# First group of the scan: zero products moved beside the updates, a bank of its own for the fourth turned block, copies in pieces, key transfers in halves

## The reference, cut to what matters

```python
def _attn_ref(q, k, v, beta):              # 4 batches, 8 heads, 768 tokens, head size 48
    k_n = k / (norm(k) + 1e-06)
    state = zeros(B, H, D, D)
    for t in range(S):
        kt, vt, bt = k_n[:, :, t], v[:, :, t], beta[:, :, t]
        y[:, :, t] = q[:, :, t] @ state
        v_old = state^T kt
        state = state + bt * outer(kt, vt - v_old)
# x = y as (3072 tokens, 384)
# _moe_ref: softmax gate, 8 Sinkhorn rounds, 8 experts: out += P[:, e] * (relu(x @ w1[e]) @ w2[e])
# _moe2_ref: h = x @ w_in; (h * cos(h)) @ w_out
```

## Time and profile before

| | before |
|---|---|
| median of three runs | 2214.7 us |
| the profiled execution's own time | 2215.68 us |
| its span | 2213.9 us |
| mean granted TensorE clock | 0.985 |
| PE busy | 2169.7 us, 98% |
| DVE, ACT, POOL busy | 46%, 32%, 23% |

### The profile page before, as it was taken

The page is one execution under the profiler, slowest core; times in us unless marked ns, Lnnn a source line. Parts: engine busy times, 40 slices in busy tenths (PEclk is TensorE's granted clock), DMA queues, the critical chain, the costliest instruction groups (busy, mean ns, idle before and its releaser), DMA issues.

```text
span 2213.9 us, 41130 instructions
## 1 busy us (share of the span) xinstructions
PE 2169.7 (98%) x15885; PEld 1793.8 (81%) x15885; DVE 1019.6 (46%) x1724; ACT 702.7 (32%) x1197; POOL 507.2 (23%) x409
## 2 busy tenths in 40 slices
PE   8798999999999999999999999999999999999999
PEld 7777778888888888888888888888888888888887
DVE  8898726432322323223223232232322347777777
ACT  4655543111111111111111111111111237666665
POOL 1000010045332322323323233232332330000000
PEclk6899999999999999999999999999999999999999
DMA  5434332021111111111111101111111100000001
GB/s 140 121 91 119 104 117 74 24 54 43 29 33 29 29 40 36 32 30 28 33 28 28 47 28 33 28 30 32 28 35 42 29 24 15 15 15 15 0 15 71
DMA packets 83116, 97.74 MB, mean 44 GB/s; under 512 B 6848, under 2 KB 68608, under 8 KB 83008
## 3 DMA queue, kind: packets, MB, share of 16 engines
q1 hardware_dynamic: 83008, 96.18, 16.0%
HBM read 82.69 MB, written 8.75 MB: 41 GB/s over the span
## 4 chain that ended last, share of the span: by engine, by line
PE 91%; DVE 6%; issue 1%; ACT 1%; DMA 0%; SPq 0%; DVEq 0%; ACTq 0%
PE h L774 7%; PE h L776 7%; PE h L775 7%; PE p_h L774 7%; PE p_h L776 7%; PE p_h L775 7%; PE am_y L812 4%; PE am_y L813 4%; PE am_y L814 4%; PE cy_y_y L812 4%; PE cy_y_y L813 4%; PE cy_y_y L814 4%; PE o_y L812 2%; PE o_y L813 2%; PE state_y L814 2%; PE state_y L812 2%
## 5 line engine op out<-in xcount | busy, mean ns | idle before, releaser
L1384 POOL TENSOR_TENSOR acc<-acc,py 128x512 f32 (+1 forms) x252 | 324.1, 1318 | 746.2 <-DVE py L1732 746.2
L1244 ACT ACTIVATE hhi<-h 128x512 fp32r<-128x512 f32 x182 | 109.0, 599 | 769.7 <-PE h L776 769.7
L1695 DVE SCALAR_TENSOR_TENSOR hlo<-h,hhi 128x512 fp32r<-128x512 f32 x182 | 125.9, 692 | 473.5 <-ACT hhi L1244 473.5
L1695 DVE SCALAR_TENSOR_TENSOR hlo<-p_h,hhi 128x512 fp32r<-128x512 f32 x182 | 125.8, 691 | 404.3 <-ACT hhi L1244 404.3
L1346 POOL TENSOR_TENSOR wlo<-stage,whi (+1 forms) x114 | 146.8, 1289 | 630.1 <-ACT whi L1089 605.2
L774 PE MATMUL p_h<-xhi,whi 128*128 (+1 forms) x690 | 269.1, 390 | 0.6 <-DVE scr L1792 0.6
L774 PE MATMUL h<-xhi,whi 128*128 (+1 forms) x690 | 268.9, 390 | 0.0
L776 PE MATMUL h<-xhi,wlo 128*128 (+1 forms) x690 | 268.7, 389 | 0.0
L776 PE MATMUL p_h<-xhi,wlo 128*128 (+1 forms) x690 | 268.7, 389 | 0.0
L775 PE MATMUL p_h<-xlo,whi 128*128 (+1 forms) x690 | 268.6, 389 | 0.0
L775 PE MATMUL h<-xlo,whi 128*128 (+1 forms) x690 | 268.6, 389 | 0.0
(11 more groups left out here) (279 smaller groups left out, 3820.6 us busy)
## 6 DMA issues: line engine op xcount, KB each, us to landing
stage<-wcat SPq DMA_DIRECT2D x38, 768.0 KB, 4.4
pb<-p_scratch SPq DMA_DIRECT2D x84, 256.0 KB, 4.7
kq<-kqt SPq DMA_DIRECT2D x48, 192.0 KB, 3.5
v<-vrow SPq DMA_DIRECT2D x24, 192.0 KB, 3.7
kb<-krow SPq DMA_DIRECT2D x24, 192.0 KB, 3.8
acc<-yT SPq DMA_DIRECT2D x144, 32.0 KB, 2.3
kT<-kta SPq DMA_DIRECT2D x20, 192.0 KB, 4.3
acc<-y_scratch SPq DMA_DIRECT2D x5, 768.0 KB, 4.7
```

What stands on the lines that cost most here:

```text
L1244: act.activation(hhi[:, j, :], hps[j % 2][:, 0:TILE], ACT.Relu).then_inc(s["hhi_done"], 1)
L1384: pool.tensor_tensor(y, y, py[:, d, :], ALU.add).then_inc(s["added"], 1)
L1695: dve.scalar_tensor_tensor(out=hlo[:, j, :], in0=hps[j % 2][:, 0:TILE], scalar=0.0, in1=hhi[:, j, :].bitcast(F32), op0=ALU.max, op1=ALU.su ...
```

## The change: what it does

- **Zero products.** Before the scan: 14 in place of 6 ahead of the first joins, and 4 in place of 2 ahead of the first turned blocks. In the steps they stood in `beside_residual`, ahead of the wait for R; now they stand behind `beside_update`, after the next step's query products: 4 in (0,0), 2 in (0,1), 3 in (0,2), 2 in (0,3), 2 in (1,0), 3 in (1,1), none in (1,2). Four more stand in (0,0) between `joins(3)` and `turned(3)`.
- **Own bank.** `turned(3)` writes `h_ps` in place of `o_ps`, no longer waits for `fixed(2)`, and moves from step (0,1) to the end of (0,0). `joined(3)` on ACT moves ahead of `first_scatter(1)`.
- **ACT order in the first group.** `first_scatter(2)` moves behind the outputs of (0,1). The key copies `products(3, ...)` move from ahead of the update copy W to behind the outputs. `extract(2)`, four pieces in one go before, is spread: one piece after (0,1), one in (0,2) before the state, two after its outputs.
- **SP.** The first half of `wraw` stays in (0,0); the second moves from (0,1) to (1,2), and its ACT split from (0,3) to (1,3). The two halves of kT for group 4, both issued in (0,2) before, are issued in (0,2) and (0,3); those for group 5, both in (1,0) before, in (1,0) and (1,1). `move_y`, which runs in odd steps, stands ahead of them.
- **DVE.** Before the scan, the mask copies and `masked(0)` move ahead of `fixed(0)`.

```diff
-UNREAD = {(0, 1): 3, (0, 2): 3, (0, 3): 3, (1, 0): 3, (1, 1): 3, (1, 2): 3}
+UNREAD = {(0, 0): 4, (0, 1): 2, (0, 2): 3, (0, 3): 2, (1, 0): 2, (1, 1): 3}
@@ SP, in the loop over the steps, behind move_y
-                if g == 0 and c < 2:
-                    load_w(0, c, wraw)
-                if (g, c) in ((0, 2), (1, 0)):
-                    for part in range(2):
-                        load_kT(AHEAD + 1 + g, part)
+                if (g, c) in ((0, 0), (1, 2)):
+                    load_w(0, g, wraw)
+                if (g, c) in ((0, 2), (0, 3)):
+                    load_kT(AHEAD + 1, c - 2)
+                if (g, c) in ((1, 0), (1, 1)):
+                    load_kT(AHEAD + 2, c)
@@ PE, turned(c)
-            if c > 0:
+            if c in (1, 2):
                 pe.wait_ge(a["zx_fixed"], c)
+            bank = h_ps if c == STEPS - 1 else o_ps
@@ PE, beside_residual
             if (g, c) == (0, 1):
-                turned(3)
                 first_merge(2)
-            if (g, c) in UNREAD:
-                pe.wait_ge(a["m_evac"], {(0, 1): 2, (0, 2): 4, (0, 3): 4, (1, 0): 6}.get((g, c), 8))
-                unread(UNREAD[g, c], am_ps[1 if (g, c) == (0, 3) else 0])
@@ PE, step
             query_products(i + 1)
             beside_update(g, c)
+            if (g, c) in UNREAD:
+                bank = {(0, 0): o_ps, (0, 1): h_ps, (0, 3): am_ps[1]}.get((g, c), am_ps[0])
+                if g == 0 and c < 2:
+                    pe.wait_ge(a["zx_fixed"], 2 + 2 * c)
+                else:
+                    pe.wait_ge(a["m_evac"], 4 if g == 0 else 6)
+                unread(UNREAD[g, c], bank)
...
                 turned(2)
                 joins(3)
+                unread(4, am_ps[1])
+                turned(3)
@@ PE, before the scan
-        unread(6, state_ps)
+        unread(14, state_ps)
...
-        unread(2, state_ps)
+        unread(4, state_ps)
@@ ACT
-                if (g, c) in KEYS_BESIDE:
+                if (g, c) in KEYS_BESIDE and g > 0:
                     ... products(...) ahead of updates(g, c)
...
                     second_merged(2)
-                    first_scatter(2)
                     first_merged(3)
+                elif (g, c) == (0, 2):
+                    extract(2, 1, 2)
@@ ACT, behind the outputs
                     second_merged(1)
+                    joined(3)
                     first_scatter(1)
-                    joined(3)
                 if (g, c) == (0, 1):
+                    first_scatter(2)
                     second_merged(3)
                     first_scatter(3)
+                    extract(2, 0, 1)
+                if (g, c) in KEYS_BESIDE and g == 0:
+                    ... products(...)
+                if (g, c) == (0, 2):
+                    extract(2, 2, 4)
-                if c == 1 and far:
+                if c == 1 and far and g > 0:
                     extract(g + 2)
-                if g == 0 and c == 3:
+                if g == 1 and c == 3:
                     for chunk in range(NT // 2, NT):
                         split_hi(0, chunk, 0, 1, wraw)
@@ DVE, before the scan
-        fixed(0)
-        leaf_start(1)
         ... mask copies
         masked(0)
+        fixed(0)
+        leaf_start(1)
         fixed(1)
```

More of the change, by code:

```diff
@@ L529, in turned @@
             pe.wait_ge(a["join_evac"], c + 1)
-            if c > 0:
+            if c in (1, 2):
                 pe.wait_ge(a["zx_fixed"], c)
+            bank = h_ps if c == STEPS - 1 else o_ps
             for n in range(HEADS):
                 for b in range(2):
-                    mm = pe.matmul(rows(o_ps, b)[:, n * HL:(n + 1) * HL], rows(join, b)[:, c * HEADS + n, :],
+                    mm = pe.matmul(rows(bank, b)[:, n * HL:(n + 1) * HL], rows(join, b)[:, c * HEADS + n, :],
                                    rows(z_x, b)[:, c * HEADS + n, HL:L], start=True, stop=True)
@@ L1180, in _ @@
                     second_merged(1)
+                    joined(3)
                     first_scatter(1)
-                    joined(3)
                 if (g, c) == (0, 1):
+                    first_scatter(2)
                     second_merged(3)
                     first_scatter(3)
+                    extract(2, 0, 1)
+                if (g, c) in KEYS_BESIDE and g == 0:
+                    key_group, m = KEYS_BESIDE[g, c]
+                    products(key_group, 2 * m)
+                    products(key_group, 2 * m + 1)
+                if (g, c) == (0, 2):
+                    extract(2, 2, 4)
                 if (g, c) in KEYS_AFTER:
@@ L1509, in fixed @@
             units = slice(c * HEADS, (c + 1) * HEADS)
+            bank = h_ps if c == STEPS - 1 else o_ps
             z = z_x[:, units, HL:L]
-            dve.tensor_tensor(z, z, o_ps[:, 0:HEADS * HL].rearrange("p (n i) -> p n i", i=HL), ALU.subtract).then_inc(a["zx_fixed"], 1)
+            dve.tensor_tensor(z, z, bank[:, 0:HEADS * HL].rearrange("p (n i) -> p n i", i=HL), ALU.subtract).then_inc(a["zx_fixed"], 1)
             dve.wait_ge(a["zx_fixed"], c + 1)
```

## The result

The changed kernel took 2230.7 us in the median (2228.7 to 2231.3, 4 runs) beside 2216.1 for the kernel before (4 runs): a ratio of 1.0062, 95% interval 1.0045 to 1.0080. Later, beside other runs of the kernel before, it took 2228.7 us (4 runs), ratio 1.0060 (1.0040 to 1.0080). So it is slower by some 13.5 us, where 6.3 were forecast and the range ended at +10.8 (2225.5). The forecast time, 2221.0, was counted from the first three runs of the kernel before (median 2214.7); with the fourth its median is 2216.1, so 1.4 us of the distance to 2230.7 lie in that base.

A forecast was written before the change was run, and what follows sets the result against it. PE is busy 98% of the span after the scan, DVE bounds up to R(0,2). +0.8 + 0 - 3.9 + 0.3 + 8.8 + 0.3 = +6.3 us on 2215.7, less 1.0 to the median: 2221.0 us; range 2210.5 to 2225.5.

The forecast's parts named there:

- Part 5: Step (1,2): key half (5,1), issued behind the y moves, lands late and PE waits; +8.8 us (+5 to +9.5).
- Rival (b): SP's queue: the y moves let key half (5,1) through in time, so step (1,2) loses nothing; 2209.4 us, chance 0.17.
- Part 3: R(0,3) to end of (0,3): W starts when the weight split ends, issue stall gone; -3.9 us (-0.5 to -4.5).
- Part 4: End of (0,3) to end of (1,1): late key half (4,1) lands when needed; 0 us (-0.5 to +1.5), plus 0.3 for the clock.
- Part 1: Up to R(0,2): zero products delay R(0,1), DVE's two idles go, clock halfway; +0.8 us (-3.6 to +2.7).
- Part 2: R(0,2) to R(0,3): the 4.2 us wait on W goes or shrinks but DVE's chain decides; 0 us (-0.5 to +0.5).
- Rival (c): Clock low all through (0,0) and (0,1), issue stall of (0,3) half kept; +10 us, 2224.8 us, chance 0.18.
- rival (a): Clock holds at full from 26 us, so the stretch up to R(0,2) gains 3.6; +1.9 us, 2216.6 us, chance 0.23.

The follow-up runs named there:

- E9: The kernel before with only the second key half of group 5 moved, to (1,1) behind the y moves; 2226.35 us, ratio 1.0038.
- E4: The kernel before with ACT's new order in the first group alone; 2219.4 us, ratio 1.0007.
- E15: The changed kernel with keys, zero products and second weight half as before; 2216.9 us, ratio 0.9997.
- E6: The changed kernel with keys and zero products as before; 2216.5 us, ratio 0.9991.
- E2: The kernel before with only the key halves of groups 4 and 5 spread as in the change, behind the y moves; 2228.8 us, ratio 1.0048.
- E10: The kernel before with only the second key half of group 4 moved, to (0,3) behind the y moves; 2219.15 us, ratio 1.0002.
- E3: The kernel before with all the zero products of the change and nothing else; 2220.8 us, ratio 1.0015.
- E5: The changed kernel with both key halves of a group issued together in (0,2) and (1,0), as before; 2221.0 us, ratio 1.0011.
- E13: The kernel before with the change's early zero products alone, up to (0,1); 2218.0 us, ratio 1.0000.
- E14: The kernel before with the change's late zero products alone, from (0,2) on; 2218.0 us, ratio 1.0002.

## Why the prediction was wrong in size and right in direction

**Part 5, right.** The forecast's 8.8 + 0.3 stands against 10.0 in the profiles and 8.4 in E9's times. Within it two terms were off and nearly cancel. The half came sooner (products at +14.0 us, forecast +15.3), since the moves started 0.7 us earlier and took 8.04 us and not 8.9. What followed took longer (9.4 us from the first key product, forecast 7.5): PE's list behind the keys runs in series and at the lower clock, where I had W on ACT as last. Rival (b) is refuted by E9: the half does not pass the moves. One reading of the forecast was wrong and did no harm: the half was not "in place long ahead before". In the kernel before its two DMAs were issued only by 106.1 us, with the half ahead of them, for which PE already waited a little (1.4 us in the second execution):

```profile
109.05 0.27 PE L471 MATMUL h<-kT 48*64 48x64 f32 x2 [0.40 <-DMA kT<-kta]
```

The Trainium skill, DMA: Bandwidth & Descriptors, section "Issuing engines are not separate DMA queues", says the time to start a DMA is usually small beside the DMA. In the two steps where a key half stood behind them, the twelve small moves took 8.0 to 10.4 us to issue, 0.7 to 0.9 each, and landed in 2.0 to 2.8 in the median: for them the time to issue is the larger of the two for the series, and a third of the DMA for each.

**Part 3, the failed step, 5.1 of the 6.9 us between the table's 13.2 and the forecast 6.3.** It said: "W starts when the weight split ends, R + 4.1 (78.97 + 1.65 - 76.54), + 0.5, then 2.7 us for lines 698 to 709". W did start at R + 4.0, but was not last. I had not priced PE's own list from R to line 698 in its new form at the lower clock: in the changed kernel 1.1 for X and R, 1.84 for the queries, 1.22 for two zero products, which part 3 did not name, 1.92 for the merge, and an issue stall of 0.92. I had also compared with one execution that held a 2.5 us issue stall; the other execution of the kernel before did the same stretch in 9.03 us, and beside that one only 1.7 of the 3.9 was there to be gained. Over all executions the gain is 10.8 - 10.7 = 0.1 us; the rest of the +1.2 of the table may be the chance of four. The times agree: E4's interval (-0.7 to +3.5) and E15's (-2.9 to +1.6) leave no room for a gain of 3.9 (E6's, -4.4 to +0.4, does). A stall of that kind moves: it is 2.5 us at line 482 in one execution, 1.3 at line 704 in the other, 2.3 at line 704 in E6.

**Part 4, mis-sized: +2.3 for +0.3.** I put keys and need at the same moment (+14.7 and +14.8), and both were off. The key products started at +16.1 in the changed kernel, +16.6 in E2 and in E10, as the moves took 9.4 to 10.4 us in these three and the half's two DMAs 1.05 to 1.8 to issue, where I had 9.0 and one step of 0.45. And PE stood ready at +14.5, +12.1 and +13.1: the +14.8 was the moment of a (1,0) that had itself lost 2.1 us at issue, and whenever (1,0) goes better, the late half takes that away. This may be the part of E2's 11.7 us that part 5 does not hold, as E10's profile suggests; E10's times leave 0 to 2.7.

**Part 1: -0.7 for +0.8**, inside its bounds. DVE's two idles went as forecast: from R(0,1) to R(0,2) it took 11.1 and 11.4 us, beside 13.2 and 13.9 before, 2.3 less. R(0,1) came 1.7 late, not 3.1. The 3.1 was a slip: halfway between 5.0 late and 1.3 early is 1.9, which would have made part 1 -0.4 and the sum +5.1. (The mean in rival (b) is also off: -2.8 and -7.2 give -5.0, not -5.3.) **Part 2: 0 for 0**, and in E4, with the 4.2 us wait gone, R(0,3) came only 0.5 earlier.

**The zero products** were mis-sized too: the forecast had +0.8 for the early ones and nothing for the rest; E3 shows 2 to 4 us for all, and E5 beside E6 shows 4.5. So by runs and not by stretches, in medians, the loss is 9.7 us for the late halves (E5), 4.5 for the zero products, and -1.4 for the rest (E6; -4.4 to +0.4), which had been forecast at -3.9 with the idles on top. The profiles put some of the zero products' time in PE's list of (0,3), where it belongs to the failed step, but E13 and E14 did not divide it.

**Rival (c)** had its issue stall half kept and reached 2224.8; its clock condition, low all through (0,0) and (0,1), was not met: from 26 to 60 us the changed kernel was granted 0.65 and 0.68, the kernel before 0.50 and 0.54. Nor was rival (a)'s, full from 26 us on. What was missing from all cases is one in which the clock stays low in (0,3): with the forecast's other terms kept, that alone turns the -3.9 into about 0, and the sum of +6.3 into about +10. In the table the rest is mostly part 4, +2.0, and part 5, +0.9.

## What to carry to other kernels

A load put behind a series of small DMAs on one issuing engine starts when the last of them has been issued: add up the issue times of all that stands ahead, and compare with the moment of need in the fastest course of the steps before, not in the one profiled. When a wait is taken away, add up the waiting engine's own list at its lower clock level too; here PE reached the reader 3.2 us after W was there, and the gain was nil. A stall that one execution shows is not a gain to be had until a second execution shows it in the same place.

## What the runs showed of the hardware that was not expected

DVE's two 64 x 64 mask copies took 1.46 us in both executions of the kernel before, where POOL's select ran beside them, and 0.38 us in both of the changed kernel, where they stand 4 us ahead of it. The other fourteen profiles agree: 1.46 or 1.47 in the nine with DVE's old order, 0.39 to 0.45 in the five with the new. The kernel before, DVE and POOL:

```profile
33.51 1.46 DVE L1581 COPY mask<-mask_all 64x64 f32<-64x64 f32 x2
...
33.66 1.26 POOL L1340 TENSOR_SCALAR_AFFINE_SELECT a_leaf<-a_leaf 128x1024 f32<-128x1024 f32 x1 [19.31 <-DVE stat L1458]
```

The changed kernel:

```profile
28.73 0.38 DVE L1596 COPY mask<-mask_all 64x64 f32<-64x64 f32 x2
...
32.83 1.26 POOL L1356 TENSOR_SCALAR_AFFINE_SELECT a_leaf<-a_leaf 128x1024 f32<-128x1024 f32 x1 [18.50 <-DVE stat L1474]
```

That the two disturb each other is what the times suggest; no run takes POOL's select away.

A busy PE did not hold the full clock: in (0,3) of the changed kernel it was granted 0.50 while busy for 9.62 of 10.95 us, in E6 0.86 while busy for 6.96 of 9.56. (Part of the higher share is the clock's own doing, since products take longer at the lower level.)
